# Attention by pairs of blocks on TensorE, with a shorter set-up and an earlier second weight cast

## What is computed

```python
scores = q @ k.T / sqrt(D)               # B=2, H=8, S=768, D=64
keep = (pos_k < 8) | ((0 <= rel) & (rel < 96))
scores = where(keep, scores - slope[h] * dist, -1e9)
a = softmax(scores); x = (a @ v) as (1536, 512)
h = x @ w_in                             # 512 -> 2048
g = P(h) / (Q(h) + 1e-6)                 # cubic over quadratic
x = g @ w_out                            # 2048 -> 512
h = x @ w2_in                            # 512 -> 1024
solu = h * softmax(h); ln = layernorm(solu) * g_ln
out = ln @ w2_out                        # 1024 -> 512
```

## Time and profile before

| | us |
|---|---|
| median of 3 runs (lowest to highest) | 511.91 (510.41 to 513.51) |
| the profiled execution, whole | 511.26 |
| its span, first to last instruction | 509.4 |

### The profile page before, as it was taken

How to read it: one execution, slowest core, us unless ns; L and a number is a source line. 1 busy time by engine, 2 the same in 40 slices (tenths; PEclk the granted TensorE clock), 3 DMA queues, 4 the chain that set the end, 5 groups by cost and what they waited for, 6 DMA issues and landing times.

```text
span 509.4 us, 7169 instructions
## 1 busy us (share of the span) xinstructions
PE 497.6 (98%) x2572; PEld 391.5 (77%) x2572; DVE 374.4 (73%) x697; ACT 272.5 (53%) x486; POOL 61.9 (12%) x129
## 2 busy tenths in 40 slices
PE   7999999988999999999999999999999999999997
PEld 6656555766888888788888888888888888888885
DVE  5667787269999978988778999989876455555550
ACT  4998889446555455645455554455253443344341
POOL 3665656230000000000000000000000000000000
PEclk9999999998999999999999999999999999999999
DMA  8998548162000000000002345422112222111201
GB/s 314 409 412 297 184 149 333 57 226 106 1 0 1 0 2 0 1 0 1 0 0 84 103 128 163 145 82 84 41 41 63 62 63 62 62 62 62 62 32 50
DMA packets 26958, 50.21 MB, mean 99 GB/s; under 512 B 2224, under 2 KB 16560, under 8 KB 25392
## 3 DMA queue, kind: packets, MB, share of 16 engines
q1 hardware_dynamic: 23760, 37.23, 21.2%
q0 software_dynamic: 2880, 12.58, 7.2%
q10 hardware_dynamic: 288, 0.01, 0.0%
HBM read 40.38 MB, written 3.15 MB: 85 GB/s over the span
## 4 chain that ended last, share of the span: by engine, by line
PE 92%; DMA 2%; DVE 2%; ACT 1%; issue 1%; POOL 1%; SPq 0%; POOLq 0%; DVEq 0%
PE ps L1039 9%; PE ps L1041 9%; PE ps L1040 9%; PE ps L979 8%; PE ps L980 8%; PE ps L981 8%; PE ps L925 5%; PE ps L1102 4%; PE ps L1104 4%; PE ps L1103 4%; PE ps L1059 4%; PE ps L1058 4%; PE ps L1057 4%; PE ps L915 4%; PE ps L940 4%; DMA k_sb<-in_k_win 2%
## 5 line engine op out<-in xcount | busy, mean ns | idle before, releaser
L1039 PE MATMUL ps<-gate_hi,bank_b_hi 128*128 128x512 f32 x192 | 75.7, 394 | 4.0 <-issue 3.5
L1040 PE MATMUL ps<-gate_lo,bank_b_hi 128*128 128x512 f32 x192 | 75.2, 392 | 0.0
L979 PE MATMUL ps<-tok_hi,bank_a_hi 128*128 128x512 f32 x192 | 75.2, 392 | 0.0
L1041 PE MATMUL ps<-gate_hi,bank_b_lo 128*128 128x512 f32 x192 | 75.2, 392 | 0.0
L980 PE MATMUL ps<-tok_lo,bank_a_hi 128*128 128x512 f32 x192 | 74.8, 390 | 0.0
L981 PE MATMUL ps<-tok_hi,bank_a_lo 128*128 128x512 f32 x192 | 74.7, 389 | 0.0
L465 ACT ACTIVATE quad<-ps 128x1024 f32<-128x1024 f32 x24 | 24.7, 1028 | 70.1 <-DVE rest L756 70.1
L393 POOL TENSOR_SCALAR probs<-probs,small 128x256 f32<-128x256 f32 (+1 forms) x96 | 48.8, 519 | 41.0 <-DVE small L633 40.7
L738 DVE SCALAR_TENSOR_TENSOR quad<-quad,small,absh 128x1024 f32<-128x1024 f32 x24 | 30.8, 1283 | 29.1 <-ACT absh L468 29.0
L427 ACT ACTIVATE probs<-negs,small 128x256 f32<-128x256 f32 (+1 forms) x96 | 46.5, 485 | 10.5 <-DVE small L623 9.6
L623 DVE CUSTOM_DVE_ANT_0 negs<-ps,bias 128x256 f32<-128x256 f32 (+1 forms) x96 | 37.9, 397 | 19.0 <-PE ps L915 18.8
(11 more groups left out here) (94 smaller groups left out, 962.2 us busy)
## 6 DMA issues: line engine op xcount, KB each, us to landing
v_sb<-in_v_win SPq DMA_DIRECT2D x8, 704.0 KB, 5.3
bank_a_raw<-in_w_in SPq DMA_DIRECT2D x4, 1024.0 KB, 11.4
bank_a_hi<-in_w_in POOLq DMA_DIRECT2D x4, 1024.0 KB, 9.0
bank_b_raw<-in_w_out SPq DMA_DIRECT2D x4, 1024.0 KB, 10.2
bank_b_hi<-in_w_out POOLq DMA_DIRECT2D x8, 512.0 KB, 7.1
q_sb<-in_q_t SPq DMA_DIRECT2D x16, 192.0 KB, 4.8
k_sb<-in_k_win SPq DMA_DIRECT2D x8, 384.0 KB, 5.7
stage_hi<-tok_hi SPq DMA_DIRECT2D x12, 256.0 KB, 2.7
```

Of the source, the lines that this page charges most:

```text
L979: pe.matmul(banks(bank, 1), bank_a_hi[:, f, ws], x_hi, start=(k == 0), stop=False)
L1039: pe.matmul(banks(4 + k, 1), bank_b_hi[:, f, ws], g_hi, start=first, stop=False)
L1040: pe.matmul(banks(4 + k, 1), bank_b_hi[:, f, ws], g_lo, start=False, stop=False)
L1041: mm = pe.matmul(banks(4 + k, 1), bank_b_lo[:, f, ws], g_hi, start=False, stop=last)
```

## The change

- TensorE takes two blocks per round: T(n), T(n+1), S(n+6), S(n+7), V(n-2), V(n-1). The scores of two blocks share a PSUM bank, and VectorE shifts them when both are there.
- ScalarE and VectorE run four blocks ahead (`AHEAD`), with 5 `probs` and 4 `probs_t` buffers; the sums and reciprocals run two ahead. Every fourth copy of transposed probabilities goes to VectorE. `tok_hi` and `tok_lo` are written a little later.
- The set-up: the global keys are handled on a 2 x 8 tile and not on 384 columns, the flag is computed by GpSimd, the scores of blocks 0 and 1, the first biases and the first shifts come ahead of the branch; 8 warm-up matmuls.
- w_in's raw loads all go among the reloads; its casts go at blocks 10, 16, 22 and 28; the splits start at block 16.
- Three of eight casts of w_out go when batch 0's last values are done (block 41), and `split_out_low(0)` goes ahead of the first polynomial. up(0) and up(1) follow the last two rounds, up(2) the last values.

The diff, cut to this:

```diff
-    PB = 4
+    PB, TB = 5, 4
...
+    def scores_of(n, h):
+        return banks(2 * (n // 2 % 2) + h, 1)[:, n % 2 * WIN:n % 2 * WIN + WIN]
...
-    AHEAD = 2
+    AHEAD, SCORES_AHEAD, SUMS_AHEAD = 4, 6, 2
+    FIRST_SCORES = 2
+    COPY_EVERY = 4
+    DONE_B0 = HEADS - BLOCKS
-    WARM_UP = 14
+    WARM_UP = 8
-    SPLIT_FROM, CAST_FROM = 14, 2
+    SPLIT_FROM, CAST_FROM, CAST_EVERY = 16, 10, 6
... (SyncE)
-        load_w_in(0)
-        load_w_in(1)
         take = windowed(sp)
         with sp.If(take == 1):
-            next_pair(1, with_w_in=True)
-            with sp.Fori(2, PAIRS) as pr:
-                next_pair(pr)
+            FREED = B * (PAIRS - 1)
+            for k in range(FREED + 1):
+                if k < FREED:
+                    sp.wait_ge(scores_ready, (k + 1) * BLOCKS)
+                    load_qk(k % B, k // B + 1)
+                if k:
+                    sp.wait_ge(values_ready, k * BLOCKS)
+                    load_v((k - 1) % B, (k - 1) // B + 1)
+                if 1 <= k <= 4:
+                    load_w_in(k - 1)
             load_w_out()
... (GpSimd)
-                i, part = divmod(n - CAST_FROM, 3)
+                i, part = divmod(n - CAST_FROM, CAST_EVERY)
                 if part == 0 and 0 <= i < 4:
                     cast_w_in(i)
+            pool.wait_ge(values_ready, DONE_B0)
+            for j in range(EARLY_OUT):
+                cast_w_out(j)
... (ScalarE)
+            if n % COPY_EVERY == COPY_EVERY - 1:
+                return
             act.wait_ge(turned_ready, n + 1)
... (VectorE)
+        def attend_copy(n):
+            if n % COPY_EVERY != COPY_EVERY - 1:
+                return
+            dve.wait_ge(turned_ready, n + 1)
...
+            dve.tensor_copy(dst, src).then_inc(turned_copied_dve, 1)
...
+        for h in range(2):
+            attend_bias(0, h, OF_FIRST)
+        dve.wait_ge(bias_ready, 2)
+        for h in range(2):
+            attend_shift(0, h)
+        for h in range(2):
+            attend_bias(0, h, OF_WINDOW)
+        dve.wait_ge(bias_ready, 4)
+        for h in range(2):
+            attend_shift(1, h)
         take = windowed(dve)
         with dve.If(take == 1):
+            for n in range(2):
+                attend_sums(n)
+                attend_shift(n + 2, 0)
+                attend_reciprocals(n)
+                attend_shift(n + 2, 1)
             for n in range(HEADS):
                 attend_unit(n)
+            attend_low(HEADS - 4)
...
+            split_out_low(0)
             gate_poly(0)
... (TensorE)
+        def attend_two(n):
+            for m in (n, n + 1):
+                attend_turn(m)
+            for m in (n + SCORES_AHEAD, n + SCORES_AHEAD + 1):
+                if m < HEADS:
+                    attend_scores(m)
             if n:
-                attend_previous(n - 1)
+                for m in (n - 2, n - 1):
+                    attend_values(m)
...
+        for n in range(FIRST_SCORES):
+            attend_scores(n)
         take = windowed(pe)
         with pe.If(take == 1):
+            for n in range(FIRST_SCORES, SCORES_AHEAD):
+                attend_scores(n)
+            for n in range(0, HEADS, 2):
+                attend_two(n)
+                if n == HEADS - 4:
+                    pe.wait_ge(shifted_ready, 2 * HEADS - 4)
+                    up(0)
+                if n == HEADS - 2:
+                    pe.wait_ge(shifted_ready, 2 * HEADS)
+                    up(1)
+            for n in (HEADS - 2, HEADS - 1):
+                attend_values(n)
+            up(2)
```

More of the change, by code:

```diff
@@ L86, in attention_feed_forwards @@
     w = WORK
-    PB = 4
+    PB, TB = 5, 4
     negs = [[at(f"negs{i}{h}", [P, WIN], F32, w + (2 * i + h) * KB) for h in range(2)] for i in range(2)]
     w += 4 * KB
[L90 to L93, removed]
+    spare = iter(range(w, WORK + 22 * KB, SLICE))
+    probs = [at(f"probs{i}", [P, 2, WIN], F32, next(spare)) for i in range(PB - 1)]
+    probs_t = {i: at(f"probs_t{i}", [P, 2 * WIN], F32, next(spare)) for i in (2, 3, 0, 1)}
+    probs += [at(f"probs{PB - 1}", [P, 2, WIN], F32, next(spare))]
+    w = WORK + 22 * KB
     NB = WIN + P
@@ L385, in cast_w_in, with cast_w_out @@
             pool.dma_start(bank_a_hi[:, tiles, :], w_in[:, tiles]).then_inc(in_hi_loaded[i], 16)
+        def cast_w_out(j):
+            tiles = slice(2 * j, 2 * j + 2)
+            pool.dma_start(bank_b_hi[:, tiles, :], w_out[:, tiles]).then_inc(outw_hi_loaded[j], 16)
+        EARLY_OUT = slot_bytes // (2 * SLICE)
         with pool.If(take == 1):
@@ L399, in _ @@
                 cast_w_in(i)
+            pool.wait_ge(heads_hi, HEADS)
+            for j in range(EARLY_OUT):
+                cast_w_out(j)
         pool.wait_ge(heads_hi, HEADS)
-        for j in range(FT // 2):
-            tiles = slice(2 * j, 2 * j + 2)
-            pool.dma_start(bank_b_hi[:, tiles, :], w_out[:, tiles]).then_inc(outw_hi_loaded[j], 16)
+        for j in range(EARLY_OUT, FT // 2):
+            cast_w_out(j)
         for j in range(FT // 2):
@@ L449, in attend_unit @@
             if k < HEADS:
[L450 to L454, removed]
+                attend_exp(k, 0)
+            if n % 3 == 0 and 6 <= n < HEADS - 3:
+                attend_out(n - 4)
+            elif n == HEADS - AHEAD:
+                attend_out(DONE_B0 - 1)
+            attend_copy(n)
             if k < HEADS:
-                attend_exp(k, k % 2, k % PB, k % BLOCKS, 1)
+                attend_exp(k, 1)
         def gate_inputs(g):
@@ L667, in attend_unit @@
                     attend_bias(pr + 1, m - (BLOCKS + 2), OF_FIRST)
-            if n + 1 < HEADS:
-                attend_reciprocals(n + 1, (n + 1) % PB)
+            if n % 3 == 1 and 7 <= n < HEADS - 3:
+                attend_low(n - 5)
+            elif n == HEADS - AHEAD:
+                attend_low(DONE_B0 - 1)
+            attend_copy(n)
             f, part = divmod(n - SPLIT_FROM, 2)
@@ L924, in attend_turn, with attend_values @@
                     c = h * WIN + half * P
-                    mm = pe.transpose(banks(4 + par, 1)[:, c:c + P], probs[pbuf][:, h, half * P:(half + 1) * P], ident[:])
+                    mm = pe.transpose(banks(4 + n % 2, 1)[:, c:c + P], probs[n % PB][:, h, half * P:(half + 1) * P],
+                                      ident[:])
             mm.then_inc(turned_ready, 1)
-        def attend_values(n, par, m, done, v_load):
-            b, i = divmod(m, BLOCKS)
+        def attend_values(n):
+            k, i = divmod(n, BLOCKS)
+            pr, b = divmod(k, B)
             if i == 0:
-                pe.wait_ge(v_loaded[b], v_load)
-            pe.wait_ge(turned_copied, n + 1)
-            if i % 3 == 0 and done is not None:
-                pe.wait_ge(heads_lo, done)
+                pe.wait_ge(v_loaded[b], 16 * pr + 16)
+            wait_copied(n)
+            if i % 3 == 0 and n >= 2 * PER_HALF:
+                pe.wait_ge(heads_lo, n - PER_HALF)
             for half in range(0 if i else 1, 2):
```

232 lines of the change are left out of this document (111 added, 121 removed).

## The result

The changed kernel takes 491.36 us (median of 4 runs, 490.98 to 491.82), the kernel before in the same comparison 512.71 (4 runs, 510.41 to 514.22): a ratio of 0.959, 95% interval 0.955 to 0.963. I had said 495, with 489.5 to 503.5 as the range that holds in 8 of 10 cases. The profiled execution took 491.82 us, its span 489.9; against the 509.4 of before that is 19.5 us less.

What follows compares the result with a forecast made beforehand. TensorE, 92% of the chain, was taken as the bound, with waits in the attention and first gate. Attention 12.8, start -1.4 and gate 5.1 make 16.5 us off 511.26: 495 us, range 489.5 to 503.5 for 8 in 10.

Steps and rivals of the forecast that it cites:

- rival 4: Attention and start: better than forecast, pace 1.48 us a block and clock up at once, 490.5 us; chance 0.08.
- Fixed cost of a group: TensorE's attention: 0.50 us a block is fixed cost of its groups; pairs save 0.25, giving 1.45 us a block.
- VectorE next: Attention from block 16: VectorE needs 1.48 us a block against TensorE's 1.45, so it is late by a hair.
- The pace: Attention: 1.54 us a block, 0.07 of it added for waits; the 82.6 us stretch becomes 69.8, gain 12.8 us.
- Set-up and clock: Start: after the shorter warm-up the clock rises in attention's first rounds; 1.4 us lost, bounds 1.5 gained, 3 lost.
- The gate: First gate: 3.7 us hole and the low clock behind it (1.4 us) go; gain 5.1 us, bounds 0 and 5.1.
- DMAs moved: w_in's raw loads go behind reloads, its casts are spread out: charged nothing, with a cover of eight blocks, 12 us.
- Rival 1: Attention: VectorE's copy and splits, or ScalarE, hold the pace near 1.65; 5 us more, 500 us; chance 0.25.
- Rival 2: Attention: fixed 0.50 us belongs to each block, not the switch; TensorE stays at 1.70; 505 us; chance 0.07.
- rival 3: First gate: its wait stays, through a late cast or a late ScalarE chain; 500 us; chance 0.08.
- Rival 5: Attention: clock stays at its low level after the short warm-up, all streaming doubles; 549 us; chance 0.05.

## Why the prediction was right, and where it was off

The forecast was 16.5 us less than the profiled execution of before; it is 19.4. The measured 491.36 lies in the range for 8 in 10, and just outside the 491.5 to 499 that the forecast had as its own: of rival 4 (pace 1.48, clock up at once) the second half came true.

- **Fixed cost of a group.** Right. Predicted 0.50 us a block, halved by pairs, 17.4 us of TensorE for twelve blocks; rounds of 3.11, 2.69 and 2.89 us, six blocks, make 8.69, so 17.4 for twelve. Single groups gave 1.81 again.
- **VectorE next.** Right in kind, priced too low: its copy has a pitch of 0.60 us as bounded, it was busy in 99% of the second half, and a copy handed to ScalarE or a split moved to another block only moved the bound. But from T(18) to T(42) a block takes 1.55 us, with VectorE busy nearly all the time, where 1.48 was worked out for it. What no row had priced is the split beside a denser GpSimd: 773 ns long on average in the changed kernel where it was 670, some 0.05 us a block.
- **The pace.** I took 1.54 us a block, 0.07 of it for waits. From T(4) to T(42) it is 57.76 / 38 = 1.52, of which 1.45 is the bare length (55.27 / 38 in the run with hardly any splits and fewer loads) and 0.07 waiting. The sum came out by two errors that offset each other in part: VectorE was dearer than priced, and ahead of block 16 there were hardly any waits. The stretch from T(0) to the first `up` is 68.7 us where 69.8 was forecast, 1.1 us better; it also holds fewer scores, as six blocks of them lie ahead of T(0) and not three, which the working did not count and which is part of the 1.1.
- **Set-up and clock.** Wrong: 1.4 us lost was forecast, 0.3 us won in the profiled execution (other executions with this start had T(0) up to 0.95 us earlier still). The step that failed is "After the shorter one TensorE has only short bursts of scores". The scores of four of the six blocks stand right behind the warm-up, from 5.24 to 8.23 us, TensorE was busy in 3.23 of the 3.30 us from 5.0 to 8.3, and full clock is recorded from 7.65 us on, where it was 7.3 before. So no round of the attention ran at the low level, and the 2 us that were charged for two such rounds fell away; from T(4) to 40 us every round had its bare length. T(0) came at 10.29 and not 10.9. And the run with one warm-up matmul had the low level up to 11.6 us and was no slower. This one term is 1.7 of the 2.9 us by which the forecast fell short; the rest is, to 0.1 us, the 1.1 above.
- **The gate.** Right: 5.1 us forecast. In the traces of the kernel before without and with the gate's part, T(42) to the first `down` is 30.20 and 26.49 us (3.7 for the hole), and from there to the end 392.63 and 391.15 (1.5 for the clock). In the changed kernel it was 86.95 to 98.32 from ScalarE's square to gate_lo, 11.4 us as worked out, done 0.6 us ahead of TensorE as stated (the working's own 12.2 and 11.4 us differ by 0.8). Alone in the kernel before it was 5.0, taken out of the changed kernel 4.2.
- **DMAs moved.** Charged at nothing, and right for this kernel: no wait for k or q in its trace. But the cover is thin. It was not in the rivals, and it is what stood next once VectorE was relieved.
- **Rivals.** Rival 1 (coupling) happened in a mild form, 2.0 us and not 5. Rival 2 is refuted by the single groups, rival 3 by the gate. Rival 5 is refuted by the changed kernel's trace, which has full clock through the attention, and by two more in which the clock rose inside it, transposes and all: at 11.6 us in the changed kernel with one warm-up matmul, and at 16.9 us in the kernel before with 8. The page of the Trainium skill that spoke against ("TensorE: Matmul & The Clock Gate", Part 4) gives for this work no warning that the runs bear out. The table "Why this matters for your kernels" on the same page of the Trainium skill, with its advice to keep TensorE busy without a break before counting on full clock, does fit the lower level at 12 us of the kernel before with 8 warm-up matmuls, where TensorE had been busy in 1.77 of the 3.30 us from 5.0 to 8.3 and in 2.01 of the next 2.70.

What stays open is how the 5.3 us that are not the pairs' divide between buffers, lead and reloads; no run took them apart. The wait for k at 38 us in the trace of before is 1.1 us of it.

## What to carry to other kernels

Read the fixed cost of a kind of matmul from two groups of different size in one timeline: where it is a third of the group, as here (0.15 to 0.20 of 0.6 us), putting two of a kind together pays at once. Add up the work of the engines that feed TensorE again first, because the gain ends at the next of them. When three resources lie within a few per cent, expect nothing from moving work between two of them, as here (491.93 and 492.05 against 491.36 us); less work per step, by spreading it over idle steps, gained 1 to 2 us. Before adding warm-up work, look whether TensorE has real work at that time that may run slowly: here one warm-up matmul did as well as eight, because the scores of six blocks came first.

## What was not expected of the hardware

- The start of the kernel before is not stable. The kernel before with the gate's part alone, with its full warm-up of 14 matmuls, lost the clock again in its sparse first rounds (stretches; the clock is the third number from the right): TensorE was busy in 1.16 of 2.70 us, with no gap over 1.1 us, and then the granted clock was 0.68 and 0.75. The trace of the kernel before, with the same start, kept full clock there.

```profile
8.30:11.00 2.70, 1.16 (x6) 0.57 (x6) 2.05 (x14) 2.41 (x10) 0.72 (x2) 1.00 1.07 420
11.00:14.00 3.00, 2.96 (x13) 1.31 (x13) 1.18 (x9) 2.47 (x9) 2.02 (x5) 0.68 1.04 433
14.00:17.00 3.00, 3.00 (x23) 1.85 (x22) 1.48 (x10) 1.94 (x8) 1.43 (x3) 0.75 1.02 418
```

- The executions of the kernel before lay up to 4.8 us apart (510.0 to 514.8 in 13 runs), those of the changed kernel 0.8. The mean granted clock goes with it: 0.996 to 0.997 in the four runs up to 511.1 us, 0.987 in the two above 514. The start is not the reason: with the gate's part alone and the same start, six runs lay within 0.6 us (505.98 to 506.53). So the spread went with the gate's part; none of the slower executions was profiled, so where their clock was low is not known.
- The clock column reads 1.00 also in stretches ahead of the trace's first record of it, such as the warm-up, whose instructions ran 0.21 us apart where a transpose of the same width takes 0.11 later. There the lengths of equal groups tell the level.
